# One kernel, attention to experts to a wide layer: in the last stage, the turns of the next group's z are spread over two down steps, and each output block signals, is copied and is stored on its own

## The reference

```python
# 1. attention, batch 2, 8 heads, 768 positions, head size 64: a window of |i-j| < 16,
#    and beside it one summary key (max) and value (mean) for each block of 32 positions
x = attention(q, k, v)                      # -> 1536 tokens x 512
# 2. one of 8 experts for each token
logits = x @ w_gate + modality_bias[modality_id]
e = argmax(logits, axis=1)
out[t] = softmax(logits)[t, e[t]] * (relu(x[t] @ w1[e[t]]) @ w2[e[t]])
# 3. a wide layer
h = maximum(x @ w_in, 0)                    # 1536 x 2048
return h * h @ w_out                        # 1536 x 512
```

## Time and profile before

| what | value |
|---|---|
| median of three runs | 581.5 us |
| all three | 580.98, 581.5, 585.26 us |
| the profiled execution's own time | 584.93 us |
| its span, first to last instruction | 583.3 us |
| mean granted TensorE clock | 0.959 |
| TensorE (PE) busy | 528.6 us, 91% |
| DVE busy | 231.2 us, 40% |
| ACT busy | 187.5 us, 32% |
| POOL busy | 82.5 us, 14% |

### The profile page before, as it was taken

The page is one execution under the profiler, slowest core; times in us unless marked ns, Lnnn a source line. Parts: engine busy times, 40 slices in busy tenths (PEclk is TensorE's granted clock), DMA queues, the critical chain, the costliest instruction groups (busy, mean ns, idle before and its releaser), DMA issues.

```text
span 583.3 us, 9324 instructions
## 1 busy us (share of the span) xinstructions
PE 528.6 (91%) x3118; PEld 420.8 (72%) x3119; DVE 231.2 (40%) x434; ACT 187.5 (32%) x353; POOL 82.5 (14%) x100
## 2 busy tenths in 40 slices
PE   7878989959999699998369999999999999999996
PEld 3557778748888578786257888877888877888884
DVE  3785675966222242711552132233223224122222
ACT  1645764216221352711522222133122223122221
POOL 4423334200400040310450000011000000000000
PEclk9889988979999979999669999999999999999999
DMA  8987872691551017152220000004000001000001
GB/s 302 270 227 259 259 241 110 224 351 39 183 179 54 36 33 309 47 234 97 77 85 1 0 1 1 1 6 138 0 0 0 0 0 72 0 0 0 0 0 72
DMA packets 19272, 56.97 MB, mean 98 GB/s; under 512 B 2352, under 2 KB 2608, under 8 KB 18480
## 3 DMA queue, kind: packets, MB, share of 16 engines
q1 hardware_dynamic: 11888, 29.57, 15.9%
q0 software_dynamic: 4768, 23.60, 11.1%
q10 hardware_dynamic: 2592, 3.49, 1.6%
HBM read 42.49 MB, written 14.16 MB: 97 GB/s over the span
## 4 chain that ended last, share of the span: by engine, by line
PE 73%; issue 3%; DVE 3%; DMA 3%; ACT 3%; ACTq 1%; POOL 1%; DVEq 0%; POOLq 0%; SPq 0%
PE psum L1497 8%; PE psum L1498 8%; PE psum L1499 8%; PE psum L1478 7%; PE psum L1479 7%; PE psum L1480 7%; PE psum L1405 4%; PE psum L1406 4%; PE psum L1407 4%; PE psum L1388 4%; PE psum L1389 4%; PE psum L1390 4%; DMA x_in<-xs_d 2%; PE psum L1415 1%; ACT W L539 1%
## 5 line engine op out<-in xcount | busy, mean ns | idle before, releaser
L1187 DVE TENSOR_TENSOR sq<-r_sb 128x512 f32<-128x512 f32 x48 | 33.2, 693 | 156.7 <-ACT r_sb L650 156.7
L650 ACT ACTIVATE r_sb<-psum 128x512 f32<-128x512 f32 x48 | 28.8, 601 | 163.1 <-PE psum L1480 163.1
L1478 PE MATMUL psum<-z_hi,W 128*128 128x512 f32 x192 | 77.1, 401 | 0.8 <-DVE z_lo L1171 0.8
L1497 PE MATMUL psum<-W,s_hi 128*128 128x512 f32 x192 | 76.2, 397 | 1.1 <-DVE s_lo L1189 1.1
L1480 PE MATMUL psum<-z_hi,W 128*128 128x512 f32 x192 | 76.7, 399 | 0.0
L1479 PE MATMUL psum<-z_lo,W 128*128 128x512 f32 x192 | 76.7, 399 | 0.0
L1498 PE MATMUL psum<-W,s_hi 128*128 128x512 f32 x192 | 75.9, 396 | 0.0
L1499 PE MATMUL psum<-W,s_lo 128*128 128x512 f32 x192 | 75.8, 395 | 0.0
L1388 PE MATMUL psum<-W,x_hi 128*128 (+1 forms) x104 | 44.1, 425 | 7.6 <-DVE W L919 5.8
L1189 DVE TENSOR_TENSOR s_lo<-sq,s_hi 128x512 fp32r<-128x512 f32 x48 | 33.3, 693 | 33.6 <-ACT s_hi L652 33.6
L1405 PE MATMUL psum<-W,h_hi 128*128 (+1 forms) x104 | 42.9, 412 | 2.0 <-DVE h_lo L927 2.0
(11 more groups left out here) (198 smaller groups left out, 715.4 us busy)
## 6 DMA issues: line engine op xcount, KB each, us to landing
raw<-in_w POOLq DMA_DIRECT2D x4, 2048.0 KB, 12.3
raw<-in_w_io POOLq DMA_DIRECT2D x4, 2048.0 KB, 10.2
v_in<-in_v SPq DMA_DIRECT2D x12, 390.0 KB, 9.9
raw<-in_w SPq DMA_DIRECT2D x8, 512.0 KB, 10.2
kT<-in_kT SPq DMA_DIRECT2D x8, 400.0 KB, 7.4
q_in<-in_q SPq DMA_DIRECT2D x12, 256.0 KB, 7.9
X<-in_vT SPq DMA_DIRECT2D x2, 1536.0 KB, 14.5
x_in<-xs_d SPq DMA_DIRECT2D x12, 256.0 KB, 2.8
```

Of the source, the lines that this page charges most:

```text
L1478: pe.matmul(bank[f % 2][:, :], wh, z_hi[:, k, :], start=(k == 0), stop=False)
L1497: pe.matmul(bank[2 + j][:, :], s_hi[f % 2][:, tok], wh, start=(f == 0), stop=False)
```

## The change

Four things are done, all in the last stage.

- `z_transpose` takes the slices to turn. Slices 0 and 1 of the next group are turned between `up(15)` and `down(14)`, slices 2 and 3 between `down(14)` and `down(15)`, each under its own condition that there is a next group.
- The semaphore `m2`, counted once for each `down`, goes. In its place `mo` is counted in `down(15)` alone, once for each block, at the block's last matmul.
- ACT and DVE wait for each of their blocks by itself before they copy it.
- SP issues one store for each block (256 KB), in the order 0, 1, 2, 3, each after that block's copy. Four landings free `o_sb`.

```diff
@@ SP
             with sp.Fori(0, GROUPS) as g:
-                for h in range(2):
-                    sp.wait_ge(sem["o_a"], g * 2 + (h + 1 + AHEAD))
-                    sp.wait_ge(sem["o_v"], g * 2 + (h + 1 + AHEAD))
-                    sp.dma_start(out_v[bass.ds(g, 1), :, 2 * h:2 * h + 2, :].rearrange("a p j n -> (a p) j n"),
-                                 o_sb[:, 2 * h:2 * h + 2, :]).then_inc(sem["out"], 16)
-                sp.wait_ge(sem["out"], (g + 1) * 32)
+                for j in range(GT):
+                    sp.wait_ge(sem["o_v" if j % 2 else "o_a"], g * 2 + (j // 2 + 1 + AHEAD))
+                    sp.dma_start(out_v[bass.ds(g, 1), :, j, :].rearrange("a p n -> (a p) n"), o_sb[:, j, :]
+                                 ).then_inc(sem["out"], 16)
+                sp.wait_ge(sem["out"], (g + 1) * (GT * 16))
                 sp.sem_inc(sem["ofree"], 1)
@@ ACT (DVE the same, with z_low, j in (1, 3), tensor_copy and o_v)
                 with act.If(g < GROUPS - 1):
                     z_high(g + 1)
-                act.wait_ge(sem["m2"], (g + 1) * KFF)
                 act.wait_ge(sem["ofree"], g + AHEAD)
                 for j in (0, 2):
+                    act.wait_ge(sem["mo"], g * GT + (j + 1))
                     act.activation(o_sb[:, j, :], bank[2 + j][:, :], ACT.Copy).then_inc(sem["o_a"], 1)
@@ PE
-            def z_transpose(g):
+            def z_transpose(g, ks):
                 pe.wait_ge(sem["scale"], g * GT + GT)
-                for k in range(KD):
+                for k in ks:
                     if k >= 2:
                         pe.wait_ge(sem["zl"], g * KD + (k - 1))
@@ in down, for each block j
                     ins = pe.matmul(bank[2 + j][:, :], s_lo[f % 2][:, tok], wh, start=False, stop=(f == KFF - 1))
-                ins.then_inc(sem["m2"], 1)
+                    if f == KFF - 1:
+                        ins.then_inc(sem["mo"], 1)
@@
                 for f in range(KFF):
                     up(g, f)
+                    if f == KFF - 1:
+                        with pe.If(g < GROUPS - 1):
+                            z_transpose(g + 1, range(2))
                     if f:
                         down(g, f - 1)
                 with pe.If(g < GROUPS - 1):
-                    z_transpose(g + 1)
+                    z_transpose(g + 1, range(2, KD))
                 down(g, KFF - 1)
```

More of the change, by code:

```diff
@@ L311, in build @@
         raw0 raw1 zfill scat_a x_t x_h x_l l1 relu ht hh hl l2 y sh sla slbv slbp yall
-        ylast wo_h wo_v wo_p scale zt zh zl m1 r sqs s_h s_l m2 o_a o_v out ofree den_ok""".split()
+        ylast wo_h wo_v wo_p scale zt zh zl m1 r sqs s_h s_l mo o_a o_v out ofree den_ok""".split()
     sem = {n: nc.alloc_semaphore("s_" + n) for n in names}
@@ L1195, in _ @@
                     z_low(g + 1)
-                dve.wait_ge(sem["m2"], (g + 1) * KFF)
                 dve.wait_ge(sem["ofree"], g + AHEAD)
                 for j in (1, 3):
+                    dve.wait_ge(sem["mo"], g * GT + (j + 1))
                     dve.tensor_copy(o_sb[:, j, :], bank[2 + j][:, :]).then_inc(sem["o_v"], 1)
```

## The result

The changed kernel takes 575.97 us (median of 7 runs, 575.33 to 578.83), the kernel before 581.57 us (7 runs, 580.98 to 585.26). The ratio of the runs compared is 0.9904, interval 0.9878 to 0.9931: 4.0 to 7.1 us less. The forecast was 577.2 us with a range from 576.0 to 581.3, so the time lies 0.03 us under its lower end; the sign, and within 1%, were as forecast.

What follows compares the result with a forecast made beforehand. TensorE's order of work was taken to bound the last stage, leaving standstills and the end to win. Turns 2.2 plus stores 2.1 made 4.3 us, from the 581.5 median to 577.2 us; range 576.0 to 581.3.

Steps and rivals of the forecast that it cites:

- The turns' order: At the two turns of z, TensorE transposes in two bursts, the first straight behind `up(15)`; waits covered by `down(14)`.
- Rival A: Turns keep their wait because ACT or DVE takes up z late; only the stores' 2.1 us won, 579.4 us; chance 0.10.
- The turns' size: Each of two turns of z gets 1.12 us shorter, 2.2 us for both, bounds 1.6 to 2.5.
- the 0.07 us for each return to `down`: On TensorE at the turns, 0.07 us added each time it goes from transposes back to `down`.
- the slack of 0.1 us: At the turn, slice 2's transposes find `z_lo(0)` ready by 0.1 us, so they do not wait.
- Signals and copies: Last stage, ACT and DVE: four waits in a group instead of two, on idle queues; nobody waits, cost 0.
- The stores: At the program's end, the last 256 KB store lands 2.1 us after issue, at 580.7 instead of 582.81: 2.1 us won.
- the other end: Alternative landing time for the last store, 2.8 us as the first 512 KB store of the end; 1.4 us won.
- Rival B: Stores queue one behind the other, 2.0 us lost at the end, about 0.2 us won in all: 581.3 us; chance 0.06.
- The added branch: TensorE's added skip in the third group, which has no next z: cost taken as 0, bound 0.2 us.
- rival C: Last stage's loop: longer code must be fetched in each lap, 5.8 us if none is covered, 583.0 us; chance 0.04.
- the bound of 4.6: Upper bound on the summed gain of turns and stores, 4.3 us forecast; the lower bound is 3.0.

Runs made afterwards that it cites:

- e5_pairs: The changed kernel with stores in pairs of blocks (512 KB), signals and copies still by block; 4.58 us from the last matmul's start to the end, one execution 580.44 us.
- e4_branch: The kernel before, its transposes in their old place but under two conditions of two slices each; 582.41 us against 582.37, ratio 1.0000.
- e10_changed: The changed kernel as it is, in a further comparison with the kernel before; 579.76 us against 582.39, ratio 0.9951.

## Why the prediction was right, and where it was not

- *The turns' order.* Right: two bursts, the first straight behind `up(15)`, no idle time of TensorE before the second. Rival A is out.
- *The turns' size.* The term was 1.12 us a turn; it measured 1.22 and 1.24. What failed is the moment at which `z_lo(1)` is ready. The forecast stands on the clock of the turn before, which begins 385.11 - 380.77 = 4.34 us later. On that clock slice 3 was to start at 389.40; it started at 384.94 + 4.34 = 389.28, 0.12 us sooner. From there to `down(15)` it is 0.50 us, as forecast (389.90 - 389.40, and 385.67 - 0.23 - 384.94). The chain of `z_hi` and `z_lo` was laid end to end, record after record, and it is not: `z_hi(0)` starts at 382.87, while the record of `s_hi(15)` lasts to 382.96, and `z_lo(0)` at 383.60, while that of `s_lo(15)` lasts to 383.68. An instruction with nothing to wait for starts some 0.08 us before its predecessor's record ends, where the forecast had it 0.03 behind. Slice 3 still waited for `z_lo(1)`, but 0.07 us instead of 0.12 (384.94 against 384.44 + 0.43). Also wrong are the 0.07 us for each return to `down`: behind the first burst there are none, since `down(14)` counts from 381.88 - 0.23 = 381.65, and the eight transposes are through at 380.77 + 0.87 = 381.64. So slice 2 was due 0.07 us sooner, and the slack of 0.1 us read for it is none: its weights waited 0.17 us, but the last matmul hid that.
- *Signals and copies.* Right: block by block, 1.4 us apart on each engine; nobody waits for them.
- *The stores.* Right in kind, and 0.1 us short: 2.21 against 2.1, with a landing of 2.0 us where `y_last` had 2.1. The nearest row was the right one; the 2.8 of the other end was the price of 512 KB and not of this stage, as e5_pairs shows. Rival B is out: four stores issued 0.6 to 0.8 us apart overlap.
- *The added branch.* Right at 0; rival C is out by e4_branch and by the queue without instruction packets.
- *The sum.* 4.3 forecast, 4.7 in the trace, above the bound of 4.6 by the end's 0.1 us, and 5.6 between the medians. The first difference is the turns' term (2 x 1.12, measured 2.46) and the stores' (2.1, measured 2.21). With 4.7 in place of 4.3 the forecast would have been 581.5 - 4.7 = 576.8 us, inside the range.
- *The range.* The step that failed is "the lower end goes 0.9 below the bound of the sum": no reason is given for the 0.9, while the spread of the executions was taken in upwards. It works both ways: with 4.1 us on average over 25 runs, the 575.97 of the first seven is a low draw, and e10_changed, a high one, is at 579.76. That the time lies just outside, by 0.03 us, is chance. What parts the executions lies ahead of the last stage. Among the three of the changed kernel it goes with the granted clock there; why the clock differs, and what parts the two of the kernel before at the same 0.95, stays open.

## What to carry to other kernels

At the end of a program count what is left to move when the last result is ready, and let everything else leave earlier: here signal, copy and store must all be split, since the late signal or the single store alone takes back nearly all of it (5.68 and 6.03 us of 6.02). Where an engine stops for a chain on two others, put work of the same engine between the two halves of the turn, and measure the slack of that chain from starts and not from records laid end to end. When a change is worth less than the spread of runs, the lengths of the stages it touches tell its size far better than the medians do, and the range for a median must hold the spread on both sides.

## What the runs showed of the hardware

- A store from SP to device memory landed after 2.0 us for 256 KB, 2.8 for 512 KB and 4.2 for 1 MB at the end of the program, as close to a line as the readings go. In the first turn, where POOL's gather moved rows at the same time, the four of 256 KB took 4.4 us (median).
- Its issue took SP 0.33 us where it stored one block and 0.37 where it stored two; the store of `y_last`, one tile of 256 KB, took 0.37 as well, so size alone doesn't set it.
- ACT and DVE started an instruction with nothing to wait for 0.08 to 0.09 us before the record of the one ahead of it ended (382.87 against 382.96, 383.60 against 383.68).
- TensorE loaded the weights of a slice that waited for `z_lo` 0.05 to 0.06 us after the record of `z_lo` ended (390.52 against 390.47, 384.94 against 384.88).
- Two executions of one program differ by up to 4.5 us ahead of the last stage (275.7 and 280.2), and the runs of the kernel before, over all comparisons, lie between 578.54 and 587.74 us.
